# Fetching a tile's exponents, keys, queries and gates earlier in the queue of a three-stage kernel, and v by itself

## The chip, the cores and the metric

One core of a Trainium2 chip. The metric is the device time of one execution in microseconds; lower is better. The core has TensorE (PE), VectorE (DVE), ScalarE (ACT), GpSimd (POOL) and SyncE (SP). In this kernel SyncE computes nothing: it issues nearly all transfers, in the order of its program.

## The reference

Three stages, one behind the other. Here only the first, the mixer, is changed: an attention with gates over 4 batches, 8 heads, 768 steps and heads of 40.

```python
for t in range(S):
    m_new = np.maximum(f_gate[:, :, t] + m, i_gate[:, :, t])
    f_stab = np.exp(f_gate[:, :, t] + m - m_new)
    i_stab = np.exp(i_gate[:, :, t] - m_new)
    C = f_stab * C + i_stab * einsum('bhd,bhe->bhde', vt, kt)
    n = f_stab * n + i_stab * kt
    h_tilde = einsum('bhde,bhe->bhd', C, qt)
    denom = np.maximum(np.abs(einsum('bhd,bhd->bh', n, qt)), 1.0)
    y[:, :, t] = sigmoid(o_gate[:, :, t]) * h_tilde / denom
```

The 3072 rows of 320 that come out go to 8 experts with a capacity each (a greedy choice over the sorted logits), and then through a dense block of two matrices with an ELU between them.

## The kernel before

The mixer takes the steps in chunks of 128: 4 batches of NCH = 6 chunks, 24 tiles in all (G), numbered g. A tile has its own set of buffers, u = g modulo RING = 3: `q_in`, `k_in`, `v_in`, `o_in`, `exp_l`, `exp_r`, `xt` and others. The six tiles of the first batch are unrolled, the other three batches are a loop of six tiles.

What an engine does for a tile:
- SyncE loads q, k, o_gate and v (`load`, L216; 160 KB each, 1024 pieces of 160 bytes), all on the tile's semaphore `tile_in`, four small transfers with the exponents (`load_exponents`, L222 and L223) and stores the tile's result (`store`, L226). Behind each third tile it fetches a piece of a later stage's weights in four transfers (`weights`, L855 and L858).
- TensorE makes, in its `body`: the product with the exponents (`exponents`, L577), the transposes of keys and queries (`gather_in`, L563, L568), then, for the tile before, the product with the state (`carried`, L621) and the addend of the state (`addend`, L604, reads v), the gate's product of tile g-3 (L648), the product with the values of the tile before (`products`, L632, reads v; it signals `h_pe`), transposes of tile g-2 (L639) and the tile's scores (L588).
- ScalarE makes the tanh of the output gate (L520, signals `th_ok`), copies kT and qT, and the exponential of W (L527).
- GpSimd weighs the keys (`kw`, L314, signals `kw_ok`) and masks W (L320).
- VectorE multiplies W with the scores, updates the state, and finishes the tile before: its last step writes `xt` (L426, signals `y_ok`), for which the store of tile g-3 must have landed (`x_stored`).

The order on SyncE is written out in `turn`. For tile n, with gp = n-3 the tile that had the buffers last, it waits for `kw_ok`, `h_pe` and `th_ok` of gp, issues the four loads, waits for `e_pe` (gp's exponents are read), issues the exponents, waits for `y_ok` of gp and issues its store. All of this stands in one queue: what is behind a wait waits too.

Waits merge with the instruction behind them where there is one that can carry them; thresholds and addresses that depend on the loop's register take register instructions on SyncE.

Of the kernel before, what the change touches and what calls it, by code (L numbers as in the profile page):

```python
# [15 lines left out]
P = 128  # L16
RING = 3
# [7 lines left out]
def build(nc, q, k, v, i_gate, f_gate, o_gate, w_gate, w1, w2, w_in, w_out, out):  # L25
    B, H, S, D = q.shape
    BH = B * H
    DM = H * D
    NCH = S // P
    G = B * NCH  # L30
# [12 lines left out]
    with ExitStack() as ctx, ExitStack() as mixer:  # L43
# [3 lines left out]
        def sb(name, shape, dt=F32):  # L47
            return mixer.enter_context(nc.sbuf_tensor(name, shape, dt))
# [4 lines left out]
        def sem(name):  # L53
            return ctx.enter_context(nc.semaphore(name))
# [34 lines left out]
        q_in = [sb(f"q_in{u}", [P, H, DP]) for u in range(RING)]  # L89
        k_in = [sb(f"k_in{u}", [P, H, DP]) for u in range(RING)]  # L90

        v_in = [sb(f"v_in{u}", [P, H, 2, VP]) for u in range(RING)]
        o_in = [sb(f"o_in{u}", [P, H, D]) for u in range(RING)]
# [25 lines left out]
        gates_in = sem("gates_in")  # L119
        wg_in = sem("wg_in")  # L120
        tile_in = [sem(f"tile_in{u}") for u in range(RING)]
        const_ok = sem("const_ok")
        pool_step = sem("pool_step")
        pads_ok = sem("pads_ok")
# [3 lines left out]
        exp_in = [sem(f"exp_in{u}") for u in range(RING)]  # L128
# [3 lines left out]
        qt_pe = sem("qt_pe")  # L132
# [3 lines left out]
        e_pe = sem("e_pe")  # L136
# [6 lines left out]
        h_pe = sem("h_pe")  # L143
# [26 lines left out]

            return t[:, bass.ds(g, 1), :].rearrange("p o (n r) -> p (o n) r", r=2).unsqueeze(3).broadcast_to([P, NP, 2, V1])

        LOADS = 4 * 16

        KD = DP + D

# [12 lines left out]
        def tile_of(b, c):  # L189
            return b * NCH + c, c % RING, b * (NCH // RING) + c // RING  # L190

        def before_it(b, c, n):

            return None if peeled(b) and b * NCH + c < n else (b, c - n)

        def states_through(b, c):
            return b * (NCH - 1) + c // NCH * (NCH - 1) + min(c % NCH + 1, NCH - 1)
# [7 lines left out]
        def peeled(g):  # L205
            return isinstance(g, int)

        @block.sync
        def _(sp):
            sp.dma_start(f_rows[:], f_gate.rearrange("b h s -> (b h) s")).then_inc(gates_in, 16)  # L210
            sp.dma_start(i_rows[:], i_gate.rearrange("b h s -> (b h) s")).then_inc(gates_in, 16)

            def load(b, c, u):
                rows = bass.ds(c * P, P)
                for src, dst in ((q, q_in[u][:, :, 0:D]), (k, k_in[u][:, :, 0:D]), (o_gate, o_in[u][:, :, :]), (v, v_in[u][:, :, 0, 0:D])):
                    sp.dma_start(dst, src[b, :, rows, :].rearrange("h t d -> t h d")).then_inc(tile_in[u], 16)  # L216

            def load_exponents(b, c, u):
                for par in range(2):
                    mine = part_rows[:, bass.ds(b * H, H), c * P:(c + 1) * P].rearrange("j (n a) t -> a j n t", a=2)[par]  # L220
                    first = par * DP
                    sp.dma_start(exp_l[u][first:first + H, :].bitcast(F32), mine[2:4]).then_inc(exp_in[u], 16)  # L222
                    sp.dma_start(exp_r[u][first + H:first + H + 2, :, :].bitcast(F32), mine[0:2]).then_inc(exp_in[u], 16)  # L223

            def store(g, u):
                sp.dma_start(x_rows[bass.ds(g * P, P), :], xt[u][:, 0:DM]).then_inc(x_stored[u], 16)  # L226

            sp.wait_ge(const_ok, 3)
            load(0, 0, 0)
            for n, (a, w) in enumerate(XK):  # L230
                sp.dma_start(wg[0:w, n, 0:E], w_gate[a:a + w, :]).then_inc(wg_in, 16)
            sp.wait_ge(rows_step, 14)
            sp.dma_start(part_rows.rearrange("j r t -> r j t"), parts[:].bitcast(F32)).then_inc(parts_out, 16)
            sp.wait_ge(parts_out, 16)
            sp.wait_ge(exp_const, 1)
            load_exponents(0, 0, 0)
            for u in range(1, RING):
                load(0, u, u)
                load_exponents(0, u, u)

            def weights(i):

                if not (peeled(i) and i < 1):
                    sp.wait_ge(pieces.ok, i)
                    sp.sem_inc(sync_turn_mixer)
                pieces.fetch_up(sp, 0, lambda r, c: w_in[r, c], i)

            weights(0)

            def turn(gp, tile, b, c, u):  # L250

                sp.wait_ge(kw_ok, states_through(*tile))
                sp.sem_inc(sync_turn_mixer)
                sp.wait_ge(h_pe, gp + 1)
                sp.wait_ge(th_ok, gp + 1)
                if b is not None:
                    load(b, c, u)
                    sp.wait_ge(e_pe, gp * 2 + 2)
                    load_exponents(b, c, u)
                sp.wait_ge(y_ok, gp + 1)  # L260
                store(gp, u)

            for j in range(NCH - RING):
                turn(j, (0, j), 0, RING + j, j % RING)
                if j == RING - 1:
                    weights(1)
            with sp.Fori(1, B) as b:
                for c in range(NCH):
                    turn(b * NCH + c - RING, before_it(b, c, RING), b, c, c % RING)
                    if c % RING == RING - 1:  # L270
                        weights(b * 2 + c // RING)
            for j in range(G - RING, G):
                turn(j, (B - 1, j - (G - NCH)), None, None, j % RING)
            for u in range(RING):
                sp.wait_ge(x_stored[u], G // RING * 16)

        @block.gpsimd
        def _(pool):
# [28 lines left out]
            def body(b, c):  # L307

                g, u, i = tile_of(b, c)
                if c < NCH - 1:  # L310
                    pool.wait_ge(tile_in[u], (i + 1) * LOADS)
                    old = before_it(b, c, RING)
# [184 lines left out]
        def _(act):  # L497
# [17 lines left out]
            def body(b, c):  # L515
                g, u, i = tile_of(b, c)
                act.wait_ge(tile_in[u], (i + 1) * LOADS)
                if not (peeled(g) and g < RING):
# [21 lines left out]
        def _(pe):  # L540
# [12 lines left out]
            def gather_in(b, c):  # L553

                g, u, i = tile_of(b, c)
                pe.wait_ge(tile_in[u], (i + 1) * LOADS)
                old = before_it(b, c, 2)
# [12 lines left out]

            def exponents(g, u, i):

                pe.wait_ge(exp_in[u], (i + 1) * LOADS)
                for par, rows in enumerate(HALVES):
                    if not (peeled(g) and g < 1):
                        pe.wait_ge(w_ok, g * 2 - 1 + par)
                    nc.tensor.matmul(pE[par], exp_l[u][rows, :], exp_r[u][rows, :, :],  # L577
                                     start=True, stop=True).then_inc(e_pe, 1)
# [12 lines left out]
            def addend(b, c):  # L591

                if c % NCH == NCH - 1:
                    return
                g, u, i = tile_of(b, c)
                pe.wait_ge(kw_ok, states_through(b, c))
                last = before_it(b, c, 1)
                if last:
                    pe.wait_ge(c_ok, states_through(*last))
                pe.wait_ge(kt_ok, g + 2)  # L600
                for n in range(NP):

                    both = v_in[u][:, 2 * n:2 * n + 2, 0, :]
                    ins = nc.tensor.matmul(pC[0:KD, n, :, :], kw[u][:, 2 * n:2 * n + 2, :].rearrange("p r d -> p (r d)")[:, 0:KD],  # L604
                                           both, start=True, stop=True)
                ins.then_inc(kw_free, 1)

            def placed(u, n, r):
                at = 4 * n + r
                return v_in[u][:, :, :, :].rearrange("p h a d -> p (h a) d")[:, at:at + 2, :]  # L610
# [13 lines left out]
            def products(b, c):  # L624

                g, u, i = tile_of(b, c)
                if not (peeled(g) and g < 1):
                    pe.wait_ge(fin_step, g * 6 - 4)
                pe.wait_ge(p_ok, g * 2 + 2)
                for n in range(NP):  # L630
                    for r in range(2):
                        ins = nc.tensor.matmul(pH[:, n, :, :], PW[u][:, r, n, :], placed(u, n, r),  # L632
                                               start=(r == 0), stop=(r == 1))
                ins.then_inc(h_pe, 1)
# [34 lines left out]
            carried(B - 1, NCH - 1)  # L669
            gate(G - 3, (G - 3) % RING, G - 1)  # L670
            products(B - 1, NCH - 1)
            pe.wait_ge(xt_ok, G - 2)
            rows_to_columns(G - 2, (G - 2) % RING)
# [1290 lines left out]
```

## Time and profile before

| what | value |
|---|---|
| time, median of 3 runs (lowest to highest) | 866.09 us (865.6 to 866.79) |
| the profiled execution | 866.72 us |
| its span, first to last instruction | 864.8 us |
| mixer | from 0 to about 205 us |
| busy share of the span: PE, DVE, ACT, POOL | 92%, 61%, 53%, 45% |
| granted TensorE clock, mean | 0.98 |

All rows shown are of the profiled execution, with times from the start of its span. An engine's busy time leaves out its waits, its register instructions and the issuing of transfers, so SyncE has no busy time at all: how full it is must be read from its timeline. In the timeline a row is the start, the length, the engine and line, the operation and what it writes and reads; "x3" merges three. SPq is SyncE's queue, and the length of a transfer there is the time that its issue takes on SyncE, not that of the transfer. In brackets stands the idle time before an instruction and what ended it.

### The profile page before, as it was taken

The numbers are of one execution on the slowest core, as the hardware profiler recorded it, in microseconds if no ns is written. First come the engines' busy times: TensorE is split into PE (matmuls) and PEld (weight loads), VectorE is DVE, ScalarE is ACT, GpSimd is POOL, SyncE is SP. The second block draws the span as 40 slices with busy tenths as digits, with TensorE's granted clock in tenths as the row PEclk, the third lists the DMA queues.
The fourth block names the chain that finished last, engine by engine and source line by source line (L and its number), as shares of the span: only waits on it lengthen the run. The fifth ranks groups of instructions, "written<-read, shape, count | busy, mean of one in ns | idle before, by whom it ended". The sixth has DMA issues, their size and how long they took to land.

```text
span 864.8 us, 17734 instructions
## 1 busy us (share of the span) xinstructions
PE 795.5 (92%) x5979; PEld 740.1 (86%) x5979; DVE 528.8 (61%) x1449; ACT 462.4 (53%) x981; POOL 392.9 (45%) x467
## 2 busy tenths in 40 slices
PE   1998899898988999999999999999999999999994
PEld 0887798887777888989989998998999899999894
DVE  6465747576765965776586487658648665542441
ACT  1544344441241765388377637827763782784673
POOL 3434434344551365166345516634560763475133
PEclk9999989999997999999999999999999999999998
DMA  3887777772341021221202122120211212031000
GB/s 63 140 139 128 130 128 128 131 123 78 111 112 45 23 81 46 59 63 51 80 26 69 44 58 67 47 81 25 74 46 51 67 51 78 25 87 40 1 1 23
DMA packets 138602, 60.94 MB, mean 70 GB/s; under 512 B 104800, under 2 KB 136800, under 8 KB 138528
## 3 DMA queue, kind: packets, MB, share of 16 engines
q1 hardware_dynamic: 136224, 52.13, 27.8%
q0 software_dynamic: 2304, 7.87, 2.9%
q8 instruction: 41, 0.67, 0.3%
q14 instruction: 33, 0.27, 0.1%
HBM read 51.72 MB, written 8.26 MB: 69 GB/s over the span
## 4 chain that ended last, share of the span: by engine, by line
PE 61%; DVE 6%; ACT 5%; issue 2%; POOL 1%; DMA 0%; ACTq 0%; POOLq 0%
PE bank L1760 7%; PE bank L1845 7%; PE bank L1761 6%; PE bank L1763 6%; PE bank L1847 6%; PE bank L1846 6%; PE bank L1765 3%; PE bank L1764 3%; PE bank L1801 2%; PE bank L1803 2%; PE bank L1802 2%; PE bank L1697 2%; PE bank L1789 1%; PE bank L1786 1%; DVE unit L1441 1%
## 5 line engine op out<-in xcount | busy, mean ns | idle before, releaser
L1178 POOL TENSOR_TENSOR gl_lo<-unit,gl_hi 128x384 fp32r<-128x384 f32 x128 | 130.6, 1020 | 273.7 <-ACT gl_hi L1635 273.6
L1845 PE MATMUL bank<-Wo_hi,gl_hi 128*128 128x320 f32 x384 | 125.3, 326 | 0.5 <-POOL gl_lo L1178 0.5
L1847 PE MATMUL bank<-Wo_hi,gl_lo 128*128 128x320 f32 x384 | 119.0, 310 | 0.0
L1846 PE MATMUL bank<-Wo_lo,gl_hi 128*128 128x320 f32 x384 | 118.8, 309 | 0.0
L1438 DVE SCALAR_TENSOR_TENSOR unit<-bank,unit 128x384 f32<-128x384 f32 x104 | 57.7, 555 | 82.7 <-ACT bank L1628 82.7
L1599 ACT ACTIVATE hid_hi<-bank 128x384 fp32r<-128x384 f32 x64 | 31.5, 492 | 131.2 <-PE bank L1765 131.2
L1616 ACT ACTIVATE unit<-bank 128x384 f32<-128x384 f32 x128 | 62.3, 487 | 59.8 <-PE bank L1765 50.7
L1760 PE MATMUL bank<-x_hi,Wi_hi 128*128 128x384 f32 x224 | 80.6, 360 | 2.4 <-DVE unit L1441 1.6
L1761 PE MATMUL bank<-x_hi,Wi_lo 128*128 128x384 f32 x224 | 75.9, 339 | 0.0
L1845 PEld LDWEIGHTS bank<-Wo_hi,gl_hi 128*128 128x128 f32 x384 | 72.7, 189 | 3.2 <-POOL gl_lo L1178 3.2
L1441 DVE TENSOR_TENSOR unit<-unit,bank 128x384 f32<-128x384 f32 x128 | 70.8, 553 | 4.4
L1846 PEld LDWEIGHTS bank<-Wo_lo,gl_hi 128*128 128x128 f32 x384 | 72.7, 189 | 0.0
L1847 PEld LDWEIGHTS bank<-Wo_hi,gl_lo 128*128 128x128 f32 x384 | 72.5, 189 | 0.0
L1619 ACT ACTIVATE unit<-unit 128x384 f32<-128x384 f32 x128 | 67.2, 525 | 4.0
L1421 DVE SCALAR_TENSOR_TENSOR hid_lo<-bank,hid_hi 128x384 fp32r<-128x384 f32 x64 | 35.4, 553 | 55.3 <-ACT hid_hi L1599 55.0
L320 POOL TENSOR_SCALAR_AFFINE_SELECT W<-W 128x512 f32<-128x512 f32 x48 | 32.9, 708 | 74.9 <-ACT W L527 74.9
L1635 ACT CAST gl_hi<-unit 128x384 fp32r<-128x384 f32 x128 | 63.9, 499 | 3.9 <-DVE unit L1441 3.8
L1763 PE MATMUL bank<-x_lo,Wi_hi 128*128 128x384 f32 x224 | 57.3, 337 | 0.0
L1628 ACT ACTIVATE bank<-unit 128x384 f32<-128x384 f32 x104 | 51.5, 495 | 3.0
L464 DVE TENSOR_TENSOR PW<-bank,W 128x512 f32<-128x512 f32 x48 | 30.9, 686 | 28.3 <-PE bank L588 28.3
L632 PE MATMUL bank<-v_in,PW 128*128 128x96 f32 x384 | 47.3, 277 | 0.0
L880 POOL TENSOR_TENSOR W_lo<-stage,W_hi 128x512 fp32r<-128x512 f32 x32 | 41.4, 1294 | 9.9 <-ACT W_hi L871 9.8
(286 smaller groups left out, 2126.4 us busy)
## 6 DMA issues: line engine op xcount, KB each, us to landing
stage<-in_moe_w_dram SPq DMA_DIRECT2D x32, 320.0 KB, 2.9
stage<-in_moe_w_dram SPq DMA_DIRECT2D x32, 256.0 KB, 2.6
stage<-in_moe_w_dram SPq DMA_DIRECT2D x96, 64.0 KB, 2.5
q_in<-in_q_dram SPq DMA_DIRECT2D x24, 160.0 KB, 3.2
k_in<-in_k_dram SPq DMA_DIRECT2D x24, 160.0 KB, 3.9
o_in<-in_o_gate_dram SPq DMA_DIRECT2D x24, 160.0 KB, 4.1
v_in<-in_v_dram SPq DMA_DIRECT2D x24, 160.0 KB, 4.0
x_rows<-xt SPq DMA_DIRECT2D x24, 160.0 KB, 1.8
```

What stands on the lines that cost most here:

```text
L1178: nc.gpsimd.tensor_tensor(gl_lo[:, b, :], ex[:, b, :], gl_hi[:, b, :].bitcast(F32), ALU.subtract).then_inc(gl_ok, 1)
L1438: nc.vector.scalar_tensor_tensor(out=ex[:, b, :], in0=exp_at(f), scalar=1.0, in1=th[:, f % 2, :], op0=ALU.add, op1=ALU.mult).then_inc(em_o ...
L1441: nc.vector.tensor_tensor(ex[:, b, :], ex[:, b, :], ring[(NF + f) % 3][:, 0:CAP], ALU.max).then_inc(g_ok, 1)
L1616: nc.scalar.activation(ex[:, b, :], ring[(NF + f) % 3][:, 0:CAP], ACT.Relu, scale=-1.0).then_inc(neg_ok, 1)
L1619: nc.scalar.activation(th[:, f % 2, :], ex[:, b, :], ACT.Tanh, scale=-0.5).then_inc(th_ok, 1)
L1635: nc.scalar.copy(gl_hi[:, b, :], ex[:, b, :]).then_inc(gl_hi_ok, 1)
L1760: nc.tensor.matmul(to, w_hi[:, c, cols], x_hi[m][:, c, :], start=(c == 0), stop=False)
L1761: nc.tensor.matmul(to, w_lo[:, c, cols], x_hi[m][:, c, :], start=False, stop=False)
L1763: nc.tensor.matmul(to, w_hi[:, c, cols], x_lo[m][:, c, :], start=False, stop=False)
L1845: nc.tensor.matmul(acc[j][:, 0:DM], gl_hi[:, f % RG, t_], Wo_hi[:, f, :], start=(f == 0), stop=False)
L1846: nc.tensor.matmul(acc[j][:, 0:DM], gl_hi[:, f % RG, t_], Wo_lo[:, f, :], start=False, stop=False)
L1847: ins = nc.tensor.matmul(acc[j][:, 0:DM], gl_lo[:, f % RG, t_], Wo_hi[:, f, :], start=False, stop=(f == NF2 - 1))
```

## The change

Four things on SyncE, and what belongs to them on the readers' side:
- v has a semaphore of its own (`values_in`) and a function of its own (`load_values`). `tile_in` counts three loads instead of four. TensorE waits for `values_in` before `addend` and before `products`.
- A turn issues the exponents first, then k, q and o_gate.
- It waits for `qt_pe`, `e_pe` and `th_ok` of tile n-3 (the buffers' readers) in place of `h_pe`. v of a tile is issued one turn later, behind a wait for `h_pe` of the tile that had its buffer.
- A tile's result is stored two turns later than before (`finished`): in turn n the store of tile n-5.

```diff
-        LOADS = 4 * 16
+        LOADS = 3 * 16
+        EXPONENTS = 4 * 16
...
-                for src, dst in ((q, q_in[u][:, :, 0:D]), (k, k_in[u][:, :, 0:D]), (o_gate, o_in[u][:, :, :]), (v, v_in[u][:, :, 0, 0:D])):
+                for src, dst in ((k, k_in[u][:, :, 0:D]), (q, q_in[u][:, :, 0:D]), (o_gate, o_in[u][:, :, :])):
                     sp.dma_start(dst, src[b, :, rows, :].rearrange("h t d -> t h d")).then_inc(tile_in[u], 16)
+
+            def load_values(b, c, u):
+                sp.dma_start(v_in[u][:, :, 0, 0:D], v[b, :, bass.ds(c * P, P), :].rearrange("h t d -> t h d")).then_inc(values_in[u], 16)
...
             load(0, 0, 0)
+            load_values(0, 0, 0)
...
             for u in range(1, RING):
+                load_exponents(0, u, u)
                 load(0, u, u)
-                load_exponents(0, u, u)
+                load_values(0, u, u)
...
                 sp.wait_ge(kw_ok, states_through(*tile))
                 sp.sem_inc(sync_turn_mixer)
-                sp.wait_ge(h_pe, gp + 1)
+                sp.wait_ge(qt_pe, gp + 1)
+                sp.wait_ge(e_pe, gp * 2 + 2)
                 sp.wait_ge(th_ok, gp + 1)
-                if b is not None:
-                    load(b, c, u)
-                    sp.wait_ge(e_pe, gp * 2 + 2)
-                    load_exponents(b, c, u)
+                load_exponents(b, c, u)
+                load(b, c, u)
+
+            def finished(gp, u):
                 sp.wait_ge(y_ok, gp + 1)
                 store(gp, u)
 
+            def next_values(gp, b, c, u):
+                sp.wait_ge(h_pe, gp + 1)
+                load_values(b, c, u)
...
             with sp.Fori(1, B) as b:
                 for c in range(NCH):
-                    turn(b * NCH + c - RING, before_it(b, c, RING), b, c, c % RING)
+                    g = b * NCH + c - RING
+                    turn(g, before_it(b, c, RING), b, c, c % RING)
+                    finished(g - 2, (c - 2) % RING)
+                    next_values(g - 1, *((b, c - 1) if c else (b - 1, NCH - 1)), (c - 1) % RING)
                     if c % RING == RING - 1:
                         weights(b * 2 + c // RING)
...
-                pe.wait_ge(exp_in[u], (i + 1) * LOADS)
+                pe.wait_ge(exp_in[u], (i + 1) * EXPONENTS)
...
                 g, u, i = tile_of(b, c)
+                pe.wait_ge(values_in[u], (i + 1) * 16)
                 pe.wait_ge(kw_ok, states_through(b, c))
...
                 pe.wait_ge(p_ok, g * 2 + 2)
+                pe.wait_ge(values_in[u], (i + 1) * 16)
```

## Rows read from the trace of the kernel before

**Rows 1.** Waits, 60 to 190 us: total, times, longest, in us.
```profile
PE bank L577 <- DMA exp_r<-part_rows: 12.0, 6, 3.0
```

**Rows 2.** Waits of SyncE's queue, 30 to 190 us, same columns.
```profile
SPq L216 <- PE bank L632: 3.0, 3, 1.9
```

**Rows 3.** Timeline of SyncE, turns of tiles 16 and 17.
```profile
131.61 0.41 SPq L216 DMA_DIRECT2D q_in<-in_q_dram  x1
132.11 0.53 SPq L216 DMA_DIRECT2D k_in<-in_k_dram  x1
132.73 0.66 SPq L216 DMA_DIRECT2D o_in<-in_o_gate_dram  x1
133.48 0.76 SPq L216 DMA_DIRECT2D v_in<-in_v_dram  x1
134.52 0.68 SPq L222 DMA_DIRECT2D exp_l<-part_rows  x1
135.40 0.28 SPq L223 DMA_DIRECT2D exp_r<-part_rows  x1
...
136.73 0.27 SPq L223 DMA_DIRECT2D exp_r<-part_rows  x1
137.20 0.40 SPq L226 DMA_DIRECT2D x_rows<-xt  x1
138.07 0.40 SPq L216 DMA_DIRECT2D q_in<-in_q_dram  x1
...
144.98 1.83 SPq L858 DMA_DIRECT2D stage<-in_moe_w_in_dram  x3
147.69 0.39 SPq L216 DMA_DIRECT2D q_in<-in_q_dram  x1
```

**Rows 4.** Timeline of TensorE, tile 16 to the start of tile 17.
```profile
138.43 0.48 PE L577 MATMUL bank<-exp_r,exp_l 64*128 64x512 f32 x2
138.84 0.66 PE L563 MATMUL bank<-ident,k_in 128*128 128x128 f32 x4
...
140.64 0.90 PE L604 MATMUL bank<-v_in,kw 128*104 128x96 f32 x8
...
145.17 0.48 PE L577 MATMUL bank<-exp_r,exp_l 64*128 64x512 f32 x2
```

**Rows 5.** Windows: length, busy time by engine, granted clock, DMA share, GB/s.
```profile
128.00:129.00 1.00, 1.00 (x12) 0.83 (x13) 0.35 (x1) 0.12 (x1) 1.00 (x2) 1.00 1.44 164
...
130.00:131.00 1.00, 0.00 (x0) 0.00 (x0) 0.92 (x2) 0.23 (x1) 0.59 (x1) 1.00 0.05 9
```

**Rows 6.** Timelines of SyncE and of TensorE, tile 21.
```profile
170.24 0.38 SPq L216 DMA_DIRECT2D q_in<-in_q_dram  x1
...
177.42 0.66 PE L563 MATMUL bank<-ident,k_in 128*128 128x128 f32 x4
```

**Rows 7.** The page's DMA issues: count, size, median us to landing.
```profile
o_in<-in_o_gate_dram SPq DMA_DIRECT2D x24, 160.0 KB, 4.1
v_in<-in_v_dram SPq DMA_DIRECT2D x24, 160.0 KB, 4.0
```

**Rows 8.** Timeline of all engines, start of tile 18.
```profile
153.67 0.47 ACT L520 ACTIVATE o_th<-o_in 128x320 f32<-128x320 f32 x1 [2.10 <-DMA v_in<-in_v_dram]
...
154.76 1.00 PE L563 MATMUL bank<-ident,k_in 128*128 128x128 f32 x4
...
154.93 0.49 DVE L426 TENSOR_TENSOR xt<-yn,rden 128x320 f32<-128x320 f32 x1
```

**Rows 9.** Line L216: issue time in ns, least, median, most; starts.
```profile
L216 SPq DMA_DIRECT2D o_in<-in_o_gate_dram x24: 531/691/1885, 8.1 to 184.4; - x24
```

**Rows 10.** Timeline of TensorE, tile 12, and the window 108 to 116.
```profile
107.61 0.79 PE L577 MATMUL bank<-exp_r,exp_l 64*128 64x512 f32 x2 [2.97 <-DMA exp_r<-part_rows]
...
116.61 0.48 PE L577 MATMUL bank<-exp_r,exp_l 64*128 64x512 f32 x2
...
108.00:116.00 8.00, 8.00 (x47) 7.50 (x47) 1.09 (x3) 2.36 (x5) 1.95 (x3) 0.63 0.65 105
```

More of the change, by code:

```diff
@@ L121, in build @@
         tile_in = [sem(f"tile_in{u}") for u in range(RING)]
+        values_in = [sem(f"values_in{u}") for u in range(RING)]
         const_ok = sem("const_ok")
@@ L253, in turn @@
                 sp.sem_inc(sync_turn_mixer)
-                sp.wait_ge(h_pe, gp + 1)
+                sp.wait_ge(qt_pe, gp + 1)
+                sp.wait_ge(e_pe, gp * 2 + 2)
                 sp.wait_ge(th_ok, gp + 1)
-                if b is not None:
-                    load(b, c, u)
-                    sp.wait_ge(e_pe, gp * 2 + 2)
-                    load_exponents(b, c, u)
+                load_exponents(b, c, u)
+                load(b, c, u)
+            def finished(gp, u):
                 sp.wait_ge(y_ok, gp + 1)
                 store(gp, u)
+            def next_values(gp, b, c, u):
+                sp.wait_ge(h_pe, gp + 1)
+                load_values(b, c, u)
             for j in range(NCH - RING):
                 turn(j, (0, j), 0, RING + j, j % RING)
+                if j > 1:
+                    finished(j - 2, j - 2)
+                if j > 0:
+                    next_values(j - 1, 0, RING + j - 1, j - 1)
                 if j == RING - 1:
@@ L268, in _ @@
                 for c in range(NCH):
-                    turn(b * NCH + c - RING, before_it(b, c, RING), b, c, c % RING)
+                    g = b * NCH + c - RING
+                    turn(g, before_it(b, c, RING), b, c, c % RING)
+                    finished(g - 2, (c - 2) % RING)
+                    next_values(g - 1, *((b, c - 1) if c else (b - 1, NCH - 1)), (c - 1) % RING)
                     if c % RING == RING - 1:
                         weights(b * 2 + c // RING)
-            for j in range(G - RING, G):
-                turn(j, (B - 1, j - (G - NCH)), None, None, j % RING)
+            next_values(G - RING - 1, B - 1, NCH - 1, (NCH - 1) % RING)
+            for j in range(G - RING - 2, G):
+                finished(j, j % RING)
             for u in range(RING):
```

## The prediction

> **What bounds the kernel now.** The change touches only the mixer, the first 205 us, so the mixer was read first. TensorE is the busiest engine of the page, so the first question was what holds it up where it is not busy. The waits of the engines between 60 and 190 us answer that: TensorE stood 12.0 us, in 6 places, before the product with the exponents (L577), because the exponents had not landed [rows 1]. The next question is why they are late. SyncE's own waits say that it is not held back by anyone: from 30 to 190 us it waited for a semaphore 3.0 us in all, three times, each time for the product with the values (L632, h_pe) [rows 2]. SyncE's timeline shows the rest: it issues without a pause. One turn (q, k, o_gate, v, four exponent transfers, one store) takes 6.46 us from q to the next q (131.61 to 138.07), and a turn with the four weight transfers behind it takes 9.62 us (138.07 to 147.69) [rows 3]. Three tiles are therefore 2 x 6.46 + 9.62 = 22.5 us of issuing. TensorE needs 6.74 us for a tile when nothing is late (138.43 to 145.17), 20.2 us for three [rows 4]. So in the mixer **SyncE's issuing sets the pace**, and TensorE pays the difference, about 2 us, at each third tile.
>
> The remaining candidate is the transfers themselves. The share of the DMA engines is 1.44 in the microsecond from 128 and 0.05 in the one from 130, while SyncE is still issuing [rows 5]: the engines run dry in each turn. They have gaps, SyncE has none.
>
> **The change part by part.** Nothing is taken off SyncE: per tile it still issues nine transfers. I work out when the data of tile 21 (the last that TensorE stands still for) can be read by TensorE's transposes, before and after. Before, turn 21 began at 170.24 and the transposes of the keys at 177.42 [rows 6], 7.2 us later.
>
> (a) *What stands ahead of a tile's loads.* In the new order turn n issues exponents and k, q, o_gate of tile n, then the store of tile n-5 and v of tile n-1. Before, the store of tile n-4 and v of tile n-1 had gone ahead of it. So two stores and one v fewer are ahead of each turn. A store costs 0.40 us and 0.21 us of register work before it (136.73 + 0.27 to 137.60), v costs 0.76 us and 0.1 us of register work [rows 3]: 2 x 0.61 + 0.86 = **-2.08 us**, once, not for each tile.
>
> (b) *The three waits for h_pe* go: the new turn waits for qt_pe, e_pe, th_ok and kw_ok of tile n-3, all done some 12 us earlier, and its h_pe is that of tile n-4. They are idle time of the queue that sets the pace: **-3.0 us** [rows 2].
>
> (c) *The order inside a turn.* Before, the exponents came last and TensorE could begin 7.2 us after the turn. Now the three loads come last. The four exponent transfers with their register work take from 134.52 to the following store's place at 137.20, 2.7 us; the loads' third issue is 1.1 us behind their first (131.61 to 132.73) [rows 3] and o_gate lands 4.1 us after its issue [rows 7]. That is 2.7 + 1.1 + 4.1 = 7.9, with the wait's hand-over 8.0 us: **+0.8 us**, once. ScalarE's tanh and GpSimd's kw wait for the same semaphore. Before they were released ahead of TensorE (tanh at 153.67, transposes at 154.76) [rows 8], now at the same moment. The tanh takes 0.47 us and the copy of kT needs the transposes anyway, so I cost this at nothing; if it were on the path it would be at most that 0.47.
>
> (d) *Register and wait instructions.* This price is not in the trace, since the new instructions aren't. One wait more (qt_pe) stands alone in each turn. The thresholds of y_ok and h_pe and v's own address may each need a register instruction, or may be found in registers of earlier turns. The nearest rows are the gaps between two transfers with one address step and without: exp_r starts 0.2 us behind exp_l's end, k 0.1 us behind q's, about 0.08 us an instruction (133.48 + 0.76 to 134.52 holds three, 0.28) [rows 3]. Bounds are one instruction (0.08 us) and four (0.34 us) a turn; below nothing is excluded, as no wait or address disappears. I take two, 0.165 us, because part of the values are those that earlier turns made. Fifteen looped turns lie before tile 21: **+2.5 us**, and **+0.2** for the three unrolled ones.
>
> (e) *Issue times.* o_gate takes 0.53 us at least and 0.69 in the median [rows 9]. If that surplus is the queue's backlog, the new spread (four small transfers between the bursts) takes some of it away. From nothing to 0.16 us a turn, 2.4 us over 15; I count nothing, and keep this gain for the lower end.
>
> Sum for tile 21: -2.08 - 3.0 + 0.8 + 2.5 + 0.2 = **-1.6 us**. Behind it TensorE has 6.74 us a tile and SyncE 6.6, so tiles 22 and 23 keep that, and the routing and the experts start from the mixer's end and are unchanged. The profiled execution took 866.72 us (span 864.8), 0.63 over the median of 866.09. 866.72 - 1.6 = 865.1, and by the median **864.5 us**.
>
> *What becomes tight.* v of tile n-1 is issued behind the store, 4.8 us + 0.6 = 5.4 us into turn n, and lands 4.0 us later [rows 7], 9.4 us into it, while the product that needs it (L604) comes 1.8 us after the transposes (138.84 is 0.4 behind 138.43; L604 at 140.64) [rows 4], at 8.0 + 1.8 = 9.8: hidden, with 0.4 us to spare. Were it late, the products behind it on TensorE's queue wait too, but only at the third tiles. The store of tile m is now issued in turn m+5; VectorE overwrites xt three tiles on. At tile 18 that write is at 154.93, against the transposes at 154.76 [rows 8]. The store queues behind the loads that land at 8.0 us and would land about half a microsecond behind them. So VectorE may wait 0.3 to 0.5 us before L426 at each third tile; behind it on VectorE stands only the scaling of the next product, which TensorE has yet to make. Price nothing.
>
> **The rivals.**
> *The transfers set the pace* (or the new register values all lie ready). Then (d) costs nothing: -2.08 - 3.0 + 0.8 = -4.3 us, 861.8. Against it stand the gaps of rows 5; for it, that o_gate takes longer to issue than its least. The Trainium skill (DMA: Bandwidth & Descriptors, "Issuing engines are not separate DMA queues") says that the time the sequencer takes to initiate a DMA is "usually small relative to the DMA itself"; by it this rival would be the likely case and the time 861.8. The trace speaks against it here: the issuing is continuous and the engines pause.
>
> *The added instructions outweigh the gain* (slower). At four instructions a turn (d) is 15 x 0.34 = 5.1: -2.08 - 3.0 + 0.8 + 5.1 + 0.2 = +1.0 us. It also widens the stall at each third tile from 22.5 - 20.2 = 2.3 to 3.3 us. After the stall of 2.97 us that ended at 107.61 the tile took 9.0 us (to 116.61), with a granted clock of 0.63 between its two levels of 1.2 and 2.4 GHz [rows 10], against 6.74. If that happens at tile 21 nothing behind it absorbs the loss, 0.9 to 2.3 us as part or all of the tile is slow. Together +1.9 to +3.3, 868.0 to 869.4. It decides from 0.27 us a turn on. For it: each turn really has a new wait, a new threshold and a second address.
>
> *The waits just change place* (the change doesn't do what it says): the exponents are early, but TensorE stands as long before the transposes, since k, q and o_gate take their place as last; the h_pe waits of SyncE were made up anyway. Then (b) falls away: +1.4 us, 867.5.
>
> **How the numbers follow.** A measurement of this kernel can tell 0.2%, 1.7 us, from no change. The forecast (one to three instructions, -2.9 to 0 us) has 0.50; it lies on both sides of that bound, 0.20 below and 0.30 inside. Transfers or cheaper issues, -3 to -5 us, 0.18. The added instructions 0.18, of which 0.14 beyond 1.7 us. The waits changing place 0.09, of which 0.04 beyond. Something at v's or the store's new place that isn't hidden 0.05, of which 0.02 beyond. Faster 0.38, same 0.42, slower 0.20. The range goes from -4.6 (861.5) to +2.2 us (868.3), leaving out the far parts of the slower cases and the clearest gain.
>
> **What would show it.** In the new profile the wait before L577 is near nothing and one of about the same size stands before the transposes (L563) at every third tile, still put down to a load; SyncE has no wait left between 30 and 190 us; three tiles take it 22.9 us; the mixer's last xt is written at about 201. If three tiles take 23.5 us or more, (d) was too small; if 22.4 or less, too large. If VectorE waits for a store by microseconds, or TensorE for v before L604, the cover of v and the store is gone. A gain of over 5 us would mean that SyncE's issuing was not the bound.

## The result and the profile after

The changed kernel took 858.07 us (857.59 to 858.63) against 866.44 us of the kernel before: ratio 0.989, interval 0.985 to 0.993. It is faster by 8 us, five times the forecast of 1.6 us, and outside the stated range. On a second and a third chip the ratios were 0.992 (0.989 to 0.995) and 0.990 (0.987 to 0.993).

| us | before | after |
|---|---|---|
| profiled execution | 866.72 | 857.59 |
| span | 864.8 | 855.9 |
| end of the mixer (last write of xt ends) | 203.0 | 200.1 |
| rest of the span | 661.7 | 655.7 |
| granted TensorE clock, mean | 0.980 | 0.988 |

So 2.9 us of the span's 8.9 lie in the mixer, and 6.0 us behind it, where the change edits nothing. The two parts are read one after the other.

*The mixer.* Waits of the changed kernel, 60 to 190 us (total, times, longest); the line that answers to [rows 1] is now at the transposes, L583, and SyncE has no wait at all in this stretch, where [rows 2] had 3.0 us:

```profile
PE bank L583 <- DMA o_in<-in_o_gate_dram: 9.8, 7, 2.3
DVE xt L446 <- DMA x_rows<-xt: 2.2, 3, 0.9
```

The timeline of its SyncE, the turns of tiles 16 and 17, answers to [rows 3]:

```profile
131.94 0.40 SPq L218 DMA_DIRECT2D k_in<-in_k_dram  x1
132.44 0.52 SPq L218 DMA_DIRECT2D q_in<-in_q_dram  x1
133.05 0.74 SPq L218 DMA_DIRECT2D o_in<-in_o_gate_dram  x1
134.00 0.59 SPq L231 DMA_DIRECT2D x_rows<-xt  x1
134.68 0.38 SPq L221 DMA_DIRECT2D v_in<-in_v_dram  x1
135.58 0.67 SPq L227 DMA_DIRECT2D exp_l<-part_rows  x1
...
138.23 0.40 SPq L218 DMA_DIRECT2D k_in<-in_k_dram  x1
...
142.40 1.82 SPq L880 DMA_DIRECT2D stage<-in_moe_w_in_dram  x3
145.31 0.70 SPq L227 DMA_DIRECT2D exp_l<-part_rows  x1
```

A turn takes 6.29 us (131.94 to 138.23), before it took 6.46. SyncE is as full as it was. From the start of tile 3's turn to that of tile 21's three tiles take 22.3 us on average (133.8 us for 18), before 22.9. Two lengths are to be seen: v takes 0.38 us to issue where it took 0.76, and the store in front of it 0.59 where it took 0.40. The tile data of tile 21 are complete at 174.59, where [rows 6] had 177.42 (timeline of TensorE, changed kernel):

```profile
173.38 0.48 PE L597 MATMUL bank<-exp_r,exp_l 64*128 64x512 f32 x2
174.59 0.66 PE L583 MATMUL bank<-ident,k_in 128*128 128x128 f32 x4 [0.72 <-DMA o_in<-in_o_gate_dram]
```

*Behind the mixer.* The expert stage gathers rows of x by index in three transfers, and TensorE transposes each. The third came late before (timeline of TensorE, kernel before), and 13 us behind it VectorE and GpSimd met (all engines, kernel before):

```profile
245.65 0.55 PE L1753 MATMUL bank<-ident,xg 128*128 128x128 f32 x3 [1.11 <-DMA xg<-x_rows,idx]
...
259.11 1.31 POOL L888 TENSOR_TENSOR W_split<-stage,W_split 128x512 fp32r<-128x512 f32 x1 [0.33 <-ACT W_split L872]
259.29 1.16 DVE L1252 TENSOR_SCALAR hi<-hi,base 128x24 f32<-128x24 f32 x1
...
261.89 0.32 PE L1709 MATMUL bank<-pick,cmp 128*128 128x32 bf16 x6 [1.33 <-DVE cmp L1261]
```

In the changed kernel the third transposes have no wait and the same VectorE instruction has 0.24 us; GpSimd's starts after it:

```profile
242.05 0.55 PE L1775 MATMUL bank<-ident,xg 128*128 128x128 f32 x3
...
255.87 0.24 DVE L1274 TENSOR_SCALAR hi<-hi,base 128x24 f32<-128x24 f32 x1
...
256.58 1.28 POOL L910 TENSOR_TENSOR W_split<-stage,W_split 128x512 fp32r<-128x512 f32 x1 [1.01 <-ACT W_split L894]
257.34 0.32 PE L1731 MATMUL bank<-pick,cmp 128*128 128x32 bf16 x6 [0.18 <-DVE cmp L1283]
```

After that, before, TensorE's granted clock fell to half for 10.2 us (from 264.15), and in the changed kernel it did not. Windows over the same work (length, busy times, granted clock, DMA share, GB/s), the first of the kernel before, the second of the changed one:

```profile
262.00:276.00 14.00, 11.87 (x84) 10.79 (x83) 6.97 (x32) 1.60 (x3) 1.69 (x2) 0.63 0.01 1
```

```profile
257.00:268.60 11.60, 9.24 (x88) 8.29 (x88) 7.36 (x33) 1.59 (x3) 2.98 (x4) 1.00 0.09 27
```

### The profile page after: what moved, and what is told of

It reads as the page before. It is cut to its first block, busy times and chain, and to the rows that moved or that the text cites. A ratio compares the mean times of both kernels' runs of the same rounds, so it can differ in the third digit from the quotient of the medians.

```text
span 855.9 us, 17769 instructions
## 1 busy us (share of the span) xinstructions
PE 791.3 (92%) x5979; PEld 737.5 (86%) x5979; DVE 528.3 (62%) x1449; ACT 461.7 (54%) x981; POOL 392.5 (46%) x467
## 4 chain that ended last, share of the span: by engine, by line
PE 62%; DVE 9%; ACT 2%; issue 1%; POOL 1%; DMA 0%; ACTq 0%; POOLq 0%
PE bank L1782 7%; PE bank L1867 7%; PE bank L1783 6%; PE bank L1785 6%; PE bank L1869 6%; PE bank L1868 6%; PE bank L1787 3%; PE bank L1786 3%; PE bank L1823 3%; PE bank L1825 3%; PE bank L1824 3%; DVE cmp L806 2%; PE bank L1719 2%; DVE unit L1463 2%; DVE unit L1460 2%; PE bank L1811 1%
## 5 line engine op out<-in xcount | busy, mean ns | idle before, releaser
L654 PEld LDWEIGHTS bank<-v_in,PW 128*128 128x128 f32 x384 | 46.2, 197 | 0.0
```

## The experiments

Two quantities are read from each profile: the end of the mixer and the rest of the span behind it. The theories: in the mixer, SyncE's issuing sets the pace (rivals: transfers, TensorE). For the rest: the old program has a late third gather and what follows from it (rivals: SyncE's new order; chance in the clock). The profiles are from several chips, and the same program's mixer ended up to 3 us apart in them; the changed kernel's four ends have a mean of 201.6.

| profile | mixer's end | rest | third gather's wait |
|---|---|---|---|
| before, four profiles | 203.0, 204.4, 204.3, 204.9 | 661.7, 664.0, 659.0, 661.3 | 1.1, 1.2, 1.0, 0.9 |
| after, four profiles | 200.1, 201.3, 203.1, 201.8 | 655.7, 656.1, 659.1, 655.3 | 0.1 or less, 0.1 in the fourth |
| e1_sync_more | 209.1 | 655.7 | 0.0 |
| e2_store_by_scalar | 193.2 | 661.1 | 0.0 |
| e3_store_late | 203.5 | 661.9 | 1.7 |
| e4_loads_first | 194.8 | 655.4 | 0.1 |
| e5_tensor_waits, e5_again | 203.9, 207.2 | 656.4, 657.1 | 0.1, 0.0 |
| e6_values_late | 199.2 | 657.0 | 0.1 |
| e7_both | 186.1 | 654.0 | 0.0 |

**More work for SyncE: e1_sync_more.**

```diff
                 sp.wait_ge(th_ok, gp + 1)
+                for _ in range(6):
+                    sp.wait_ge(const_ok, 3)
+                    sp.sem_inc(sync_turn_mixer)
                 load_exponents(b, c, u)
```

> The changed kernel with six more instructions on SyncE in each turn (a wait that is long fulfilled, with a count), about 0.08 us each, 0.5 us a turn. If SyncE's issuing sets the mixer's pace, the turns of the 15 looped tiles up to tile 21 take 7 us more and the last write of xt moves from 200.1 to about 207. If the transfers or TensorE set the pace, SyncE has 0.5 us a turn to spare and it stays within 1 us of 200.1. For the rest of the span (from the last write of xt to the end: 661.8 us before, 655.8 after): if the missing 6 us come of what the change does to the order, it stays at 655.8; if they hang on the moment at which the routing starts, it can be anything from 655 to 662.

The mixer ended at 209.1, 9.0 us later (867.0 us by the runs). The turn went from 6.30 us (129.28 to 135.58 in the changed kernel) to 6.70 (timeline of SyncE):

```profile
135.17 0.67 SPq L227 DMA_DIRECT2D exp_l<-part_rows  x1
...
141.87 0.67 SPq L227 DMA_DIRECT2D exp_l<-part_rows  x1
```

0.40 us a turn gives 7 us over 18 turns; the other 2 are within the spread from profile to profile. TensorE's wait for the loads grew from 9.8 to 16.2 us (60 to 190 us). SyncE had nothing to spare: it sets the pace. And with a mixer that ended six microseconds later than before's, the rest of the span was still 655.7, so it doesn't hang on the moment at which the routing starts.

**Less work for SyncE: e2_store_by_scalar.** ScalarE issues the stores, each behind the exponentials of W:

```diff
-                    finished(g - 2, (c - 2) % RING)
...
+                if not (peeled(g) and g < RING):
+                    store(g - RING, u)
```

> The changed kernel with the 24 stores issued by ScalarE, behind its exponentials, in place of SyncE. SyncE loses about 0.6 us a turn: three tiles 22.0 - 1.9 = 20.2 us, as much as TensorE needs. If SyncE's issuing sets the pace the mixer ends some 5 us earlier, its last xt at about 195, and the wait of TensorE before the transposes falls from 9.8 us to under 4. If the transfers set the pace, the same bytes go, and it stays at 200. The rest of the span: 655 to 662 by the theory that it hangs on the moment, 655.8 by the theory that it is the change's.

The mixer ended at 193.2, 6.9 us earlier (expected: some 5); TensorE's wait for the loads in the same stretch fell from 9.8 to 5.3 us. The median was 852.4 us, ratio to before 0.983 (0.979 to 0.987). Its rest was 661.1, with an on-time gather, so an on-time gather alone doesn't fix the rest: this profile had four slow-clock stretches of 3.4 us behind the mixer (the one that ends every profile left out), where the changed kernel's first had one. v now stands right behind o_gate again, and its issue is back at 0.69 us in the median (issue in ns, least, median, most):

```profile
L221 SPq DMA_DIRECT2D v_in<-in_v_dram x24: 414/686/2128, 8.8 to 179.9; - x24
```

**The late stores alone: e3_store_late.**

```diff
+
+            def finished(gp, u):
                 sp.wait_ge(y_ok, gp + 1)
                 store(gp, u)
...
+                    finished(b * NCH + c - RING - 2, (c - 2) % RING)
```

> The kernel before, with only the stores moved: the result of tile n-5 instead of n-3 is stored in turn n, behind the exponents. Two stores less stand ahead of each tile's loads, 1.2 us once; nothing else changes, three waits for h_pe stay. By the queue theory the last xt comes at 201.8 instead of 203.0. If the early fetch of v's companions is what counts, nothing happens. The rest of the span: 661.8 if that part is the other edits' doing, anything from 655 to 662 if it hangs on the moment.

Nothing was gained: mixer's end 203.5, time ratio 1.001 (0.998 to 1.004). The waits for h_pe took 3.9 us, within the 3.0 to 4.1 of the four profiles of before. It may be that what SyncE has done early it waits for at the next h_pe, but this one profile doesn't show it:

```profile
SPq L216 <- PE bank L637: 3.9, 4, 1.9
```

**The order inside the turn: e4_loads_first.**

```diff
-                load_exponents(b, c, u)
                 load(b, c, u)
+                load_exponents(b, c, u)
```

> The changed kernel with k, q and o_gate issued ahead of the exponents again. In a turn the last thing that TensorE needs are then the exponents, which land 1.2 us behind their issue, not o_gate with nearly 4: data are complete 7.2 instead of 8.0 us into the turn. By the queue theory the mixer gains 0.8 us, last xt at 199.3; TensorE waits before L577's line again. If the order matters in itself (exponents early let ScalarE go ahead), it loses up to 2 us. The rest of the span as in the other runs.

The expected 0.8 us became 5.3 us in this one profile: the mixer ended at 194.8, and the runs' median was 854.5 us (ratio 0.988, 0.984 to 0.992). The store is issued behind the exponents now and costs 0.39 us, v behind it costs 0.40 (timeline of SyncE):

```profile
130.06 0.27 SPq L228 DMA_DIRECT2D exp_r<-part_rows  x1
130.54 0.39 SPq L231 DMA_DIRECT2D x_rows<-xt  x1
131.03 0.40 SPq L221 DMA_DIRECT2D v_in<-in_v_dram  x1
```

From the start of tile 3's turn to that of tile 21's all issues together took 94.4 us here, 98.5 in the changed kernel and 99.9 before. Of the 4.1 us between this and the changed kernel 4.6 us are the stores' (6.3 against 10.9), less some small ones the other way. By the profiles the change's own new order, with the exponents early, thus costs more than it gives. The times of the runs don't decide it: 0.988 has an interval that overlaps those of the changed kernel (0.989, 0.992 and 0.990).

**v by itself alone: e6_values_late.** e4 with each store again three tiles behind, and ahead of v:

```diff
-                    finished(g - 2, (c - 2) % RING)
+                    finished(g, c % RING)
```

> The changed kernel with k, q, o_gate ahead of the exponents and each store again in the turn of tile n-3, in front of v of tile n-1: what is left of the change is v by itself behind store, and the buffers' own readers in place of h_pe. If the mixer's gain comes of v standing apart (0.38 to 0.40 us to issue in place of 0.75) and of the h_pe waits gone, the last xt comes at 195 to 197 as in e4 (194.8). If the late stores carry a part, it comes 1.2 us later than in e4 at least, or the wait for y_ok comes back.

Mixer's end 199.2, time 857.65 us, ratio 0.987 (0.984 to 0.991): the changed kernel's gain or a little more, but 4.4 us behind e4. So the late stores, worth nothing alone, are worth something in the new order. The wait for y_ok is back, and with that for h_pe it makes 4.8 us, where e4 had 0.5 (waits of SyncE, 30 to 190 us):

```profile
SPq L231 <- DVE xt L445: 2.9, 3, 1.4
SPq L221 <- PE bank L653: 1.9, 5, 0.8
```

**TensorE's program alone: e5_tensor_waits.** The kernel before, with

```diff
                 g, u, i = tile_of(b, c)
+                pe.wait_ge(tile_in[u], (i + 1) * LOADS)
                 pe.wait_ge(kw_ok, states_through(b, c))
...
                 pe.wait_ge(p_ok, g * 2 + 2)
+                pe.wait_ge(tile_in[u], (i + 1) * LOADS)
```

> The kernel before, with SyncE's program untouched; only TensorE has a second, long fulfilled wait for tile_in at the two places where the changed kernel waits for values_in. That gives TensorE's program the length that it has in the changed kernel. The mixer stays as before (last xt at 203). What is told apart is the 6 us behind the mixer. Theory: they hang on when a 16 KB piece of program code is fetched by the DMA engines, since before and in e3 it falls into the third gather of the experts' rows (which lands 1.1 to 1.7 us late, and a slow-clock stretch follows) and in all kernels with the changed TensorE program it does not. Then here the gather is on time, the rest of the span is 655 to 657 us, and the time falls by 4 to 6 us without any change to the mixer. Rival: the rest hangs on SyncE's order or on chance; then it stays at 661 to 662 and the time at that of before.

The rest of the span was 656.4 us, as expected, and the gather on time. The expected 4 to 6 us of time did not come: 866.5 us against 868.4, ratio 0.998 (0.995 to 1.001), which can't be told from no change; the profile is of the fastest of the ten runs. So the kernel was measured again on another chip.

> The kernel before with TensorE's second waits, five rounds. If the late third gather and what follows it are what the rest of the span gained, this kernel is 2 to 4 us faster than before with an interval that leaves out 1, its gather is on time and there is no slow-clock stretch between 235 and 290 us. If it is chance, it is within 1 us of before and its rest is as wide.

Here the ratio was 0.994 (0.992 to 0.996), 863.5 against 868.2 us. Rest 657.1, third gather without a wait, VectorE's step 0.24 us (timelines of TensorE and of VectorE):

```profile
249.00 0.55 PE L1755 MATMUL bank<-ident,xg 128*128 128x128 f32 x3
...
262.83 0.24 DVE L1254 TENSOR_SCALAR hi<-hi,base 128x24 f32<-128x24 f32 x1
```

Two waits that wait for nothing thus gave 4.6 us on one chip, with SyncE's program untouched, and 1.9 us that are within the noise on another. The mixer's end did not gain: at 207.2 it came 2 to 4 us later than in the profiles of before.

Every run has its mean granted clock on record, and half speed can cost at most the span times what the clock lacks to 1. That is 17.3 us in the mean of the 13 runs of before on this chip (clock 0.9800) and 13.4 in the 8 of e5_again (0.9845): 4.0 us of the 4.5 between their mean times. On the chip of e5's first run it is 2.0 us of 2.3. By this estimate nearly all that TensorE's waits gain is time with the clock at its upper level.

> The changed kernel, five rounds on the same chip as the one with TensorE's waits alone. Its distance to that kernel is what SyncE's order is worth: 2.4 us by the mixers' ends of three profiles each. If it is 5 us or more, the order also keeps the clock up behind the mixer.

On the same chip the changed kernel took 860.2 us, ratio 0.990 (0.987 to 0.993): 3.4 us less than TensorE's waits alone. On the chip of e5's first run the same two kernels were 5.6 us apart (860.8 and 866.5). What the clock can account for taken off in the same way, SyncE's order is worth 3.6 and 2.5 us; the mean mixer's end moved by 2.6 from before to the changed kernel.

**Repeats.**

> The changed kernel once more, on the same chip as the others: its time beside theirs, and a second profile. The mixer's last xt should again be at 200 within 1 us if that is the mechanism's and not chance's, and the rest of the span between 655 and 658, with the third gather on time.

> The kernel before, a second profile. Told apart is what in the first one's last 661.7 us is the program's and what is chance's. If the code fetch theory holds, the third gather again lands over a microsecond late, VectorE's 24-column step takes over 1.1 us instead of 0.24 and the rest of the span is 661 to 662. If the slow-clock stretches are chance, the gather is late again, but the stretches lie elsewhere and the rest is anything from 656 to 664. The mixer ends at 203 within 1 us either way.

> The kernel before, a third profile, with the same expectations as the second: late gather by the code fetch theory every time; by chance's theory slow-clock stretches at other places and a rest of the span between 656 and 664.

> The changed kernel, a third profile. By the code fetch theory the gather is on time and the rest of the span at 655 to 657; by chance's theory the rest spreads as widely as before's. The mixer's last xt between 199.5 and 202.

> The kernel before, a fourth profile: third gather late by 1 to 1.3 us, VectorE's step behind it held up to about 1 us, mixer's end at 203 to 204.5. The slow stretch near 265 us is there if it belongs to the late gather, as in two of three profiles so far; by chance it would be at another place.

Several of these expectations missed: the rest of before was 659.0 and 664.0 where 661 to 662 stood, the changed kernel's third profile had its mixer's end at 203.1 and its rest at 659.1, and the ends of before's last three, 204.3 to 204.9, were over 1 us from the first's 203.0. What held is the gather. It was late in all four profiles of before and in e3, five of five with the old TensorE program, and in none of the eleven with more waits in it. VectorE's step took 0.92 to 1.23 us in the five, 0.24 in the eleven. In e2 the step behind it met GpSimd's product and took 1.23, and no slow stretch followed for 40 us, so that meeting alone doesn't bring one.

The slow stretches are less tied. Between 235 and 290 us there was one in four of the five late profiles (264, 266, 239 and 266 us), in none of the eleven others. But the one at 239 lies 11 us ahead of that profile's late gather, so only three of five follow it. The clock as a whole is what differs. Behind the mixer and ahead of the last stretch before's four profiles had 13.7 us at half clock in the mean, the changed kernel's four 5.1. Half of the difference, 4.3 us, is most of the 5.0 between their rests. With half of the slow time taken off, the rest is 653.6 to 654.7 us in all eleven profiles with an on-time gather, and 653.2 to 656.8, mean 655.1, in the five with a late one: the late gather and the held step themselves cost about 1 us by this estimate. Mixer's ends spread by 2 to 3 us in the same program, 203.0 to 204.9 and 200.1 to 203.1.

**Both ideas: e7_both.** Stores by ScalarE (e2) and loads first (e4).

> Stores issued by ScalarE and k, q, o_gate ahead of the exponents, else the changed kernel. If SyncE's issuing still set the pace in both, their gains add: e2 ended its mixer at 193.2 and e4 at 194.8, together 188 to 190. If TensorE's own 6.74 us a tile bound from there on, 24 tiles can't end before about 190, and one finds that its waits for loads are near nothing.

The mixer ended at 186.1, below the 188 to 190 expected and the 190 that I took for TensorE's own bound. The median is 846.7 us (841.8 to 855.8), ratio to before 0.979 (0.972 to 0.985): the fastest version measured. The profile is of the fastest of the four runs and has no slow stretch before the kernel's last microseconds (mean clock 0.996); the others' clocks are 0.994, 0.987 and 0.981. TensorE's wait for loads is nearly gone (waits, 60 to 185 us):

```profile
PE bank L593 <- DMA exp_r<-part_rows: 1.4, 2, 0.8
```

## Why the prediction was wrong

**What bounds the mixer** was right: e1, e2 and e7 move its end by what they add to or take from SyncE's issuing. The new wait stood where it was said, before the transposes (9.8 us where 12.0 stood before the exponents), SyncE lost its waits, and the mixer's end moved by 2.9 us in the first pair of profiles and 2.6 in the mean of four, against 1.6 forecast. Term by term, for the first pair:

- (b) 3.0 us of h_pe waits went, as said.
- (d) was mis-sized. From the start of tile 3's turn to that of tile 21's SyncE has 354 instructions that issue nothing, before 347: seven more, not two a turn. All time outside the issues, less the waits, went from 34.8 to 35.3 us: +0.5. In that sum stand (d)'s +2.7 and the 0.52 us of register work that (a) takes away, so **(d) was +1.0 instead of +2.7**. v's issue, for one, needed a single register step in 15 of the 18 looped turns and a second in three. The prediction's own sign of a (d) that is too large, 22.4 us or less for three tiles, came: 22.3.
- (a) and (e) took the length of an issue for the transfer's own, and it wasn't. Between the same two starts v's issues fell from 13.9 to 6.9 us, and the stores' rose from 7.1 to 10.9 (16 in place of 18), the weights' first ones from 2.4 to 4.3. All issues together went down by 1.4 us, where (a) without its register work had 1.56. That the two agree is luck: two stores and one v fewer, and a shorter v, were made up by longer stores.
- (c) was +0.5 (174.59 - 166.95 = 7.6, less 7.2), not +0.8. The turn of tile 21 itself began 3.3 us earlier, at 166.95, and not 3.9, since the turn of tile 3 began 0.65 us later (33.19 against 32.54), which no term of the sum had. -1.4 - 3.0 + 0.5 + 0.65 + 0.5 = -2.8 us is what the tile data gained.
- *What becomes tight*: VectorE waited for the store three times, 2.2 us in all, somewhat longer than the 0.3 to 0.5 us each that were forecast. v was in time in this profile, but the 0.4 us to spare were not always enough: in the changed kernel's third and fourth TensorE waited for it once, 0.5 and 0.7 us.

The **step that failed** is the last one of the sum: "the routing and the experts start from the mixer's end and are unchanged". They weren't: -6.0 us in the first pair, -5.0 in the mean of four (661.5 to 656.5). The sum put the effect of the two new waits in TensorE's program, and of the clock behind the mixer, at nothing. e5 shows that two more waits a tile in TensorE's program, with SyncE's order as before, bring the rest down to 656.8 us in the mean of two profiles, and the time by 4.6 us on one chip (1.9, within the noise, on another). Of the 8 us some 3 are the change's purpose and the larger part of the others is this by-product, most of it time that TensorE no longer spends at half clock. The prediction's sign that a gain of over 5 us would mean that SyncE's issuing was not the bound was wrong for the same reason: it took the mixer for the only place where the time could move.

How the two waits act is only partly shown; that it is by the length of TensorE's program is a guess, since no run gave it a third length or made it longer by anything but waits. In the kernel before, the only other transfer among the third gather's is a piece of program code (DMA in the window 243 to 244.9 us):

```profile
q0 software_dynamic: 47, 0.16, 32.2%
q8 instruction: 1, 0.02, 3.8%
```

In the five late profiles this packet of 16 KB starts between 0.15 us ahead of the third gather's first packet and 0.7 us behind it, takes 0.96 to 1.3 us, and two or three of the gather's 48 packets come 0.8 to 1.6 us behind the others. In the eleven others it starts 4.1 to 4.9 us ahead of the third gather. In the changed kernel it is in the window 235.5 to 237.5:

```profile
q1 hardware_dynamic: 169, 0.22, 39.4%
q8 instruction: 1, 0.02, 4.5%
```

That this packet delays the gather fits all sixteen profiles, but no run moved it by itself. That the late gather in turn brings VectorE and GpSimd together at 259 us is the timeline's order of events. Why the new program spends less time at half clock stays open, and a late gather was followed by a slow stretch in only three of five profiles. Part of a single pair's difference in the rest is the spread of such stretches from execution to execution: 655.3 to 659.1 us in the changed kernel alone.

Of the rivals, the one with transfers as the bound gave 861.8 and the nearest number. Its first reason was wrong, e1 speaks against it; its second, that the new register values lie ready, is close to what (d) measured. The Trainium skill's sentence (DMA: Bandwidth & Descriptors, "Issuing engines are not separate DMA queues") that a sequencer's time to initiate a DMA is usually small relative to the DMA itself fits a single load of 160 KB here: 0.38 to 0.76 us to issue, 3.2 to 4.1 us in the median to landing. It doesn't make the issuing cheap: nine transfers on one queue took 6.3 us in a tile of 6.7. What the same section says, that issuing from another engine saves that time, is what e2 and e7 measure: 6.9 us of the mixer against the changed kernel, 8.7 against e4.

## What to carry to other kernels

Where one queue issues everything, add up its issues and register instructions for a tile and set that against the busiest engine's tile. If it is more, the queue's own waits and issues are what counts: three waits were worth 3 us, one edit to the look-ahead alone nothing (e3), and moving the stores to another engine some 7 us of the mixer (e2). And take several profiles of both kernels, with the clock of each run, before a difference far from the edit is explained: here up to 4.6 of the 8 us came with two waits in TensorE's program that wait for nothing there.

## What the runs showed of the hardware

- The time that SyncE spends on an issue went with what it had issued just before. v's 160 KB in 1024 pieces took 0.76 us in the median right behind o_gate (before), 0.38 behind the store (changed kernel); the store 0.40 us behind the small exponents, 0.56 behind o_gate.
- A 24-column step of VectorE that takes 0.24 us took 0.92 to 1.23 while GpSimd ran a product of 1.3 us. The same step some 60 us later took 1.06 to 1.25 us in all sixteen profiles, each time with GpSimd at work.
- Waits that are long fulfilled, added to TensorE's program alone, made the kernel 4.6 us faster on one chip (ratio 0.992 to 0.996) and 1.9 us, not clear of the noise, on another; a gather 40 us behind the edited loop no longer came late.
- One and the same program had mean granted clocks of 0.973 to 0.985 in 15 runs on one chip, with times of 873.8 to 864.0 us (kernel before).
